# Attention and two dense layers on one core: two-pass values, factors by DMA, a new order of the engines

## The chip, the cores and the metric

One core of one Trainium2 chip runs the whole program. The metric is the device time of one execution in microseconds. Three runs of the kernel before gave a median of 1122.53 us (1120.88 to 1122.81). Engines are named as in the profile: PE is TensorE, DVE is VectorE, ACT is ScalarE, POOL is GpSimd, SP is the engine that issues the DMAs.

## What is computed

Attention with a memory over 4 batches x 8 heads, 576 positions, 64 columns a head, then two dense layers over the 2304 tokens. All inputs are fp32.

```python
B, H, S, D = q.shape                      # 4, 8, 576, 64
scores = scale * np.matmul(q, k.transpose(0, 1, 3, 2))
scores = np.where(causal, -1000000000.0, scores)
a = np.exp(scores - scores.max(-1, keepdims=True))
a /= a.sum(-1, keepdims=True) + 1e-09
local = np.matmul(a, v)
q_p = phi(q)                              # where(x > 0, x, exp(x) - 1) + 1
mem_ret = np.einsum('bhsd,bhde->bhse', q_p, M_prev)
mem_norm = np.einsum('bhsd,bhd->bhs', q_p, z_prev)[..., None] + 1e-06
g = 1.0 / (1.0 + np.exp(-beta))[None, :, None, None]
attn = g * mem_ret / mem_norm + (1 - g) * local
...
h = x @ w_in;  y = np.where(h > 0, h, np.exp(np.minimum(h, 0)) - 1) @ w_out
h = y @ w_in2; out = (h * np.clip(h + 3, 0, 6) / 6) @ w_out2
```

## The kernel before, in words

**Tiling.** Two heads make a pair; there are 16 pairs. The 576 queries of a head are four tiles of 128 and a last one of 64; the last tiles of both heads share one tile of 128 rows. `scores` (L370) writes the scores of query tile i for both heads, `max_rows` (L730) takes their minimum on DVE (the scores are negated), `exp_rows` (L546) the exponentials with their sums on ACT. The order of tiles is 4, 3, 2, 1, 0 (`ORDER`, L24). Then `turn` (L399) transposes the probabilities on PE in ten chunks: G (the last tile), C00 to C11 (key tiles 0 and 1 of each head), C2, C3, RMAIN (the row factors), PHI and TAIL. The chunks go through a ring of two PSUM banks (`ring_at`, L150; `chunk_free`, L390).

**High and low parts.** Products keep their precision by splitting each fp32 operand into a rounded `fp32r` part and the rest. ACT rounds a chunk (`round_chunk`, L564), DVE subtracts (`split_chunk`, L741) to give `pt_lo`. `times_v` (L439) then multiplies in three passes: high x high, low x high, high x low; the values of each head stand in a 128-column stationary tile in which the other head's 64 columns are zero. `times_m` (L454) adds the memory product for both heads at once, again in three passes. All of it accumulates in one output area (`X_AT`, L153).

**Factors.** The row sums and norms give 1/sum and the gate (`row_stats` L781 on DVE, `factors` L325 on POOL). The attention factors are laid over all partitions by nine broadcast transposes (L428, L436), copied by ACT into `r_rows` (L570, L591, L592), and `store_x` (L791) multiplies the output by them on DVE. The memory factors scale `phi` on POOL (`scale_phi` L335). `phi` of q is made in two DVE steps (L771, L774) and one exponential on ACT.

**Order.** Each engine has an order written out by hand as a loop over g (L501, L646, L830): the scores of pair g are interleaved with the turns of pair g-1. Counting semaphores are shared by all tasks of a kind (`pt_lo_done`, `pv_done`, `turned`), so that a wait counts positions in that order. `load_qk` and `load_nat` on SP bring the inputs two pairs ahead.

**Layers.** A chunk of 384 tokens goes through 16 hidden tiles: `hidden` (L463), the activation (`exp_tile` on ACT, `activate` L804 on DVE), `output` (L477). The weights are rounded on ACT (`hi_weights`) and split on POOL (`lo_weights` L293) during the first chunk. In the kernel before the first hidden tiles are mixed into the last pair (L518), and one weight tile is split in the attention stage.

## Time and profile before

| | before |
|---|---|
| median of three runs | 1122.53 us |
| the profiled execution's own time | 1122.92 us |
| its span, first to last instruction | 1121.1 us |
| PE busy (modelled ends) | 1076.2 us, 96% |
| DVE, ACT, POOL busy | 677.8, 298.4, 192.5 us |
| mean granted clock of PE | 0.993 |

The attention stage takes somewhat more than a quarter of the span, the two layers the rest. The busy shares above are means over both. Ends of matmuls are modelled in the trace, so the distance between starts is the better measure of what one costs. "Granted clock" is the share of full speed that PE was given: 1.0 is 2.4 GHz, 0.5 is 1.2 GHz.

### The profile page before, as it was taken

Reading aid. Unit: us, or ns where it says so; the run is one execution under the profiler, and the core shown is the slowest. Engines: PE = TensorE matmul, PEld = TensorE weight load, DVE = VectorE, ACT = ScalarE, POOL = GpSimd, SP = SyncE. Lnnn points to the kernel's source line nnn. Section 1 sums busy time; section 2 is a strip of 40 time slices with the busy share of each in tenths; the row PEclk is TensorE's granted clock in tenths of the full one; section 3 lists DMA queues with packets and bytes.
Section 4 is the critical chain, followed back from the end, with each engine's and each line's share of the span. In section 5 each row is a group of like instructions: output and inputs, shape, how many; then the busy total and the mean of one; then the engine's idle time right before and its main releaser. Section 6 shows DMA issues by size and latency. Waiting matters only on the chain.

```text
span 1121.1 us, 16386 instructions
## 1 busy us (share of the span) xinstructions
PE 1076.2 (96%) x6080; PEld 966.3 (86%) x6080; DVE 677.8 (60%) x1278; ACT 298.4 (27%) x737; POOL 192.5 (17%) x202
## 2 busy tenths in 40 slices
PE   5999999999889999999999999899999999999998
PEld 2667676676879999999999999898999999899997
DVE  5676766767388544545454468865656565565654
ACT  3666666666432212112121123301001010000100
POOL 3434434344265000000000025500000000000000
PEclk9999999999889999999999999999999999999999
DMA  4322121220134000000000014100000000000000
GB/s 162 119 97 101 52 101 56 98 101 20 38 113 132 1 1 1 0 0 0 0 0 0 0 37 131 57 1 13 15 0 28 0 28 0 0 28 0 28 0 28
DMA packets 16599, 44.56 MB, mean 40 GB/s; under 512 B 1968, under 2 KB 1968, under 8 KB 16560
## 3 DMA queue, kind: packets, MB, share of 16 engines
q1 hardware_dynamic: 16560, 44.05, 11.3%
q8 instruction: 23, 0.38, 0.1%
q14 instruction: 16, 0.13, 0.0%
HBM read 39.33 MB, written 4.72 MB: 39 GB/s over the span
## 4 chain that ended last, share of the span: by engine, by line
PE 89%; DVE 6%; issue 3%; ACT 1%; DMA 1%; SPq 0%; DVEq 0%
PE ps L473 35%; PE ps L494 18%; PE ps L486 17%; PE ps L450 8%; PE ps L384 3%; DVE pt_lo L751 2%; PE ps L379 1%; PE ps L459 1%; PE ps L428 1%; PE ps L418 1%; PE ps L387 1%; DVE x_all L795 1%; ACT r_rows L570 1%; PE ps L405 1%; DVE h_hi L824 1%
## 5 line engine op out<-in xcount | busy, mean ns | idle before, releaser
L473 PE MATMUL ps<-x_hi,w 128*128 128x384 f32 x1536 | 392.5, 336 | 0.0
L473 PEld LDWEIGHTS ps<-x_hi,w 128*128 128x128 f32 x1536 | 280.9, 189 | 7.4
L473 PE MATMUL ps<-x_lo,w 128*128 128x384 f32 x768 | 258.3, 336 | 0.0
L486 PE MATMUL ps<-h_hi,w 128*128 128x384 f32 x768 | 196.6, 336 | 6.0 <-DVE h_lo L826 6.0
L494 PE MATMUL ps<-w,h_hi 128*128 128x512 f32 x576 | 179.2, 392 | 3.1 <-DVE h_lo L826 3.1
L824 DVE CAST h_hi<-act_tmp 128x384 fp32r<-128x384 f32 x192 | 108.9, 567 | 100.9 <-PE ps L486 53.2
L486 PEld LDWEIGHTS ps<-h_hi,w 128*128 128x128 f32 x768 | 139.5, 189 | 7.0 <-DVE h_lo L826 7.0
L473 PEld LDWEIGHTS ps<-x_lo,w 128*128 128x128 f32 x768 | 144.7, 188 | 0.0
L296 POOL TENSOR_TENSOR w<-stage,w 128x1024 f32 (+1 forms) x32 | 77.7, 2436 | 358.3 <-ACT w L544 358.3
L486 PE MATMUL ps<-h_lo,w 128*128 128x384 f32 x384 | 129.0, 336 | 0.0
L494 PEld LDWEIGHTS ps<-w,h_hi 128*128 128x128 f32 x576 | 106.8, 188 | 22.1 <-issue 2.4
L633 ACT ACTIVATE e_act<-ps 128x384 f32<-128x384 f32 x96 | 47.2, 492 | 288.3 <-PE ps L473 288.3
L826 DVE TENSOR_TENSOR h_lo<-act_tmp,h_hi 128x384 fp32r<-128x384 f32 x192 | 113.5, 591 | 6.7
L817 DVE TENSOR_SCALAR act_tmp<-ps 128x384 f32<-128x384 f32 x96 | 53.4, 556 | 99.9 <-PE ps L473 99.9
L494 PE MATMUL ps<-w,h_lo 128*128 128x512 f32 x288 | 113.7, 395 | 0.0
L811 DVE TENSOR_SCALAR act_tmp<-e_act 128x384 f32<-128x384 f32 x96 | 38.8, 404 | 109.7 <-ACT e_act L633 108.3
L610 ACT ACTIVATE x_hi<-x_all 128x384 fp32r (+1 forms) x48 | 21.2, 513 | 300.3 <-PE ps L473 299.9
L560 ACT ACTIVATE prob<-ps,neg_max 128x512 f32<-128x512 f32 (+3 forms) x128 | 66.6, 531 | 24.7 <-DVE neg_max L739 24.7
L486 PEld LDWEIGHTS ps<-h_lo,w 128*128 128x128 f32 x384 | 72.6, 189 | 0.0
L739 DVE TENSOR_REDUCE neg_max<-ps 128x2 f32<-128x1024 f32 (+1 forms) x64 | 52.4, 819 | 32.3 <-PE ps L387 32.2
L450 PE MATMUL ps<-pt_hi,v_hi 128*128 128x128 f32 (+2 forms) x192 | 63.8, 332 | 2.9 <-DVE x_all L795 2.9
L494 PEld LDWEIGHTS ps<-w,h_lo 128*128 128x128 f32 x288 | 54.0, 187 | 11.5
(110 smaller groups left out, 1233.8 us busy)
## 6 DMA issues: line engine op xcount, KB each, us to landing
nat<-nat_in SPq DMA_DIRECT2D x16, 768.0 KB, 5.4
qk<-qk_t SPq DMA_DIRECT2D x16, 608.0 KB, 3.8
stage<-w_in SPq DMA_DIRECT2D x32, 256.0 KB, 2.7
stage<-w_out SPq DMA_DIRECT2D x32, 256.0 KB, 2.9
out<-rows_out SPq DMA_DIRECT2D x18, 256.0 KB, 2.1
beta_sb<-beta SPq DMA_DIRECT2D x1, 4.0 KB, 6.5
```

Source lines behind the costliest of these rows:

```text
L296: pool.tensor_tensor(tile[:, 1], stage[:, r], tile.bitcast(F32)[:, 0], ALU.subtract).then_inc(w_split, 1)
L450: mm = pe.matmul(ps[:, X_AT + lo:X_AT + hi], v_tile(v, u, a, t), blocks(pt, a, t, lo, hi), start=(a == 0 and t == 0 and part == 0), stop=F ...
L473: mm = pe.matmul(ps[:, bank:bank + CHUNK], w[:, n, wp, 0, cols], xp[:, m, :], start=(m == 0 and part == 0), stop=(m == KM - 1 and part == 2))
L486: mm = pe.matmul(ps[:, Y_AT + 512 * m:Y_AT + 512 * m + CHUNK], w[:, n, wp, 1, cols], hp[:, n % 2, :], start=(n == 0 and part == 0), stop=( ...
L494: mm = pe.matmul(ps[:, Y_AT + 512 * m:Y_AT + 512 * m + DM], hp[:, n % 2, rows], w[:, n, wp, 1, :], start=(n == 0 and part == 0), stop=(n = ...
L560: ex = act.activation(rows_of(u, i, a), ps[:, at:at + WIDTH[i]], ACT.Exp, bias=neg_max[:, u, x:x + 1], scale=-1.0, accum_out=stats[:, u, x ...
L633: act.activation(e_act[:, n % 2, :], ps[:, 512 * (n % 4):512 * (n % 4) + CHUNK], ACT.Exp).then_inc(h_exp_done, 1)
L739: dve.tensor_reduce(neg_max[:, u, 2 * i:2 * i + 2], rows, AX_X, ALU.min).then_inc(max_done, 1)
L811: dve.tensor_scalar(tmp, e_act[:, n % 2, :], 1.0, -1.0, ALU.min, ALU.add).then_inc(e_free, 1)
L817: dve.tensor_scalar(tmp, h, 3.0, 0.0, ALU.add, ALU.max).then_inc(act_step, 1)
L824: dve.tensor_copy(h_hi[:, n % 2, :], tmp).then_inc(h_hi_done, 1)
L826: dve.tensor_tensor(h_lo[:, n % 2, :], tmp, h_hi.bitcast(F32)[:, n % 2, :], ALU.subtract).then_inc(h_split, 1)
```

## The change

The attention stage is rewritten; the loops of the layers stay as they are, but for the start of the first chunk.

- **Values and memory in two passes.** The stationary tile of a head now holds the high part of its values in 64 columns and the low part in the other 64 (`v_split`, `m_split`), and it is multiplied with `pt_hi` and `pt_lo`. The output rows 0 to 63 and 64 to 127 are then two partial results of one head, each head has a bank of its own (`x_at`), and the first 128 queries have a bank in the ring (Q0, `first_rows`). ACT copies the lower partial results to SBUF (`low_rows`, `low_first`), DVE adds them to the upper ones into `x_all` (`sum_x`, `sum_first`), POOL multiplies by the factors (`store_x`).
- **Factors.** One transpose of a 9-column tile, one small ACT copy, a DMA to a DRAM buffer and four DMAs that load it back broadcast over 64 partitions each.
- **Phi** of q is the larger of q + 1 (now on POOL, `phi_line`) and min(exp q, 1) (DVE); one DVE step goes.
- **Semaphores:** one for each kind of task (`scored[i]`, `low_done[c]`, `rounded[c]`, `turned[c]`, `pv_done[t]`).
- **A new order on all engines** over g, with the pairs in the order of batches. The last pair's chunks use the banks of the scores (`LAST_BANKS`). Three weight tiles are rounded and split during the attention stage, and `nat` and `phi_exp` move to where the layers' tiles lie.

The diff, cut to its core:

```diff
+G, C00, C01, C10, C11, C2, R, C3, PHI, TAIL = range(10)
+Q0 = 10
+RING = (G, Q0, C00, C01, C10, R, C11, C2, C3, PHI, TAIL)
+LAST_BANKS = {C00: 5, C01: 0, C10: 1, C11: 2, C2: 3, C3: 4, R: 3, PHI: 5, TAIL: 2}
+LAST_BEFORE = {C00: G, C3: Q0, R: C2, PHI: C00, TAIL: C11, Q0: C3}
...
+            def spread_r(p):
+                sp.wait_ge(rounded[R], p + 1)
+                sp.dma_start(r_dram[p % 2], r_turned[0:2 * FULL + 1, :]).then_inc(r_sent, 16)
+                sp.wait_ge(r_sent, 16 * (p + 1))
+                if p >= 1:
+                    sp.wait_ge(x_stored, p)
+                for a in range(2):
+                    main = r_dram[p % 2, FULL * a:FULL * a + FULL].rearrange("i q -> (i q)").rearrange("(o x) -> o x", o=1)
+                    tail = r_dram[p % 2, 2 * FULL:2 * FULL + 1, REST * a:REST * a + REST]
+                    sp.dma_start(r_rows[D * a:D * a + D, 0:EDGE], main.to_broadcast([D, EDGE])).then_inc(r_loaded, 16)
+                    sp.dma_start(r_rows[D * a:D * a + D, EDGE:S], tail.to_broadcast([D, REST])).then_inc(r_loaded, 16)
...
+            for g in range(3, PAIRS + 4):
+                if is_pair(g - 4):
+                    spread_r(g - 4)
+                if 9 <= g < 9 + EARLY:
+                    load_weights(g - 9 + STAGES)
+                if is_pair(g - 1):
+                    load_qk(g - 1)
+                    load_nat(g - 1)
...
+            def store_x(p):
+                at = x_all_at(p)
+                x = x_all[:, at:at + S]
+                pool.wait_ge(x_summed, p + 1)
+                pool.wait_ge(q0_summed, p + 1)
+                pool.wait_ge(r_loaded, 64 * (p + 1))
+                pool.tensor_tensor(x, x, r_rows[:, :], ALU.mult).then_inc(x_stored, 1)
...
+            for g in range(2, PAIRS + 3):
+                if is_pair(g - 6):
+                    store_x(g - 6)
+                if is_pair(g - 5):
+                    scale_phi(g - 5)
+                if is_pair(g - 3):
+                    phi_line(g - 3)
+                if is_pair(g - 4):
+                    low_vm(g - 4)
+                if is_pair(g - 3):
+                    phi_by_z(g - 3)
+                if 5 <= g < 5 + EARLY:
+                    lo_weights(w[:, g - 5], g - 5, g - 5)
+                if is_pair(g - 2) and g >= 3:
+                    scale_q(g - 2)
+                if is_pair(g - 3):
+                    round_vm(g - 3)
+                if is_pair(g - 4):
+                    factors(g - 4)
+            scale_phi(PAIRS - 2)
+            low_vm(PAIRS - 1)
+            store_x(PAIRS - 3)
+            factors(PAIRS - 1)
+            scale_phi(PAIRS - 1)
+            lo_weights(w[:, EARLY], EARLY, EARLY)
+            store_x(PAIRS - 2)
+            store_x(PAIRS - 1)
...
+                elif c == R:
                     pe.wait_ge(r_ready, p + 1)
...
+                    mm = pe.transpose(ps[0:2 * FULL + 1, at:at + P], r_nat[:, u, 0:2 * FULL + 1], ident[:, :])
...
+            def first_values(p, a):
+                u = p % 2
+                if a == 0:
+                    pe.wait_ge(low_done[C00], p + 1)
                     pe.wait_ge(vm_split, p + 1)
                     if p >= 1:
...
+                        pe.wait_ge(x_summed, p)
+                else:
+                    pe.wait_ge(low_done[C01], p + 1)
+                for part, pt in enumerate((pt_hi, pt_lo)):
+                    mm = pe.matmul(ps[:, x_at(a):x_at(a) + S - P], v_tile(u, a, 0), blocks(pt, a, 0, P, S), start=(part == 0), stop=False)
+                mm.then_inc(pv_done[0], 1)
+            def times_v(p, t):
+                u = p % 2
+                if t < LAST:
+                    pe.wait_ge(low_done[(C11, C2, C3)[t - 1]], p + 1)
                 for a in range(2):
...
+                    for part, pt in enumerate((pt_hi, pt_lo)):
+                        mm = pe.matmul(ps[:, x_at(a) + P * t - P:x_at(a) + S - P], v_tile(u, a, t), blocks(pt, a, t, P * t, S), start=False, stop=False)
+                mm.then_inc(pv_done[t], 1)
             def times_m(p):
                 u = p % 2
...
+                pe.wait_ge(low_done[TAIL], p + 1)
+                for part, ph in enumerate((phi_t_hi, phi_t_lo)):
+                    for a in range(2):
+                        d = slice(D * a, D * a + D)
+                        mm = pe.matmul(ps[:, x_at(a):x_at(a) + S - P], m_tile(u, a)[d], ph[d, P:S], start=False, stop=(part == 1))
+                mm.then_inc(memory_done, 1)
+            def first_rows(p):
+                u, at = p % 2, ring_at(p + 1, Q0)
+                chunk_free(p + 1, Q0)
+                for a in range(2):
+                    for part, pt in enumerate((pt_hi, pt_lo)):
+                        pe.matmul(ps[:, at + P * a:at + P * a + P], v_tile(u, a, 0), blocks(pt, a, 0, 0, P),
+                                  start=(a == 0 and part == 0), stop=False)
+                for part, ph in enumerate((phi_t_hi, phi_t_lo)):
+                    for a in range(2):
+                        mm = pe.matmul(ps[:, at + P * a:at + P * a + P], m_tile(u, a), ph[:, 0:P], start=False, stop=(a == 1 and part == 1))
+                mm.then_inc(q0_done, 1)
...
+            for g in range(2, PAIRS + 2):
+                if is_pair(g - 3):
+                    turn(g - 3, G)
+                    scores(g - 3, 0)
+                if is_pair(g - 4):
+                    times_m(g - 4)
+                if is_pair(g - 2):
+                    scores(g - 2, 4)
+                if is_pair(g - 4):
+                    first_rows(g - 4)
+                if is_pair(g - 3):
+                    turn(g - 3, C00)
+                if is_pair(g - 2):
+                    scores(g - 2, 3)
+                if is_pair(g - 3):
+                    turn(g - 3, C01)
+                    turn(g - 3, C10)
+                if is_pair(g - 2):
+                    scores(g - 2, 2)
+                if is_pair(g - 3):
+                    first_values(g - 3, 0)
+                    first_values(g - 3, 1)
+                    turn(g - 3, R)
+                    turn(g - 3, C11)
+                if is_pair(g - 2):
+                    scores(g - 2, 1)
+                if is_pair(g - 3):
+                    turn(g - 3, C2)
+                    turn(g - 3, C3)
+                if is_pair(g - 3):
+                    times_v(g - 3, 1)
+                    turn(g - 3, PHI)
+                    times_v(g - 3, 2)
+                    turn(g - 3, TAIL)
+                    times_v(g - 3, 3)
+                    times_v(g - 3, 4)
+            last = PAIRS - 1
+            turn(last, G)
+            scores(last, 0)
+            times_m(last - 1)
+            first_rows(last - 1)
+            turn(last, C00)
+            turn(last, C01)
+            turn(last, C10)
+            turn(last, C11)
+            turn(last, C2)
+            first_values(last, 0)
+            turn(last, C3)
+            first_values(last, 1)
+            times_v(last, 1)
+            turn(last, R)
+            turn(last, PHI)
+            times_v(last, 2)
+            turn(last, TAIL)
+            pe.wait_ge(low_done[C01], PAIRS)
+            hidden(0, 0, 0)
+            times_v(last, 3)
+            times_v(last, 4)
+            pe.wait_ge(low_done[C10], PAIRS)
+            hidden(0, 1, 0)
+            times_m(last)
+            first_rows(last)
+            pe.wait_ge(low_done[TAIL], PAIRS)
+            hidden(0, 2, 0)
...
+            def low_rows(p):
+                act.wait_ge(memory_done, p + 1)
+                heads = ps[D:P, x_at(0):x_at(0) + 1024].rearrange("p (a q) -> p a q", a=2)
+                act.activation(x_low[D:P, :, P:S], heads[:, :, 0:S - P], ACT.Copy).then_inc(x_low_done, 1)
+            def low_first(p):
+                at = ring_at(p + 1, Q0)
+                act.wait_ge(q0_done, p + 1)
+                act.activation(x_low[D:P, :, 0:P], ps[D:P, at:at + 2 * P].rearrange("p (a q) -> p a q", a=2), ACT.Copy).then_inc(q0_low_done, 1)
...
+            def sum_x(p):
+                at = x_all_at(p)
+                dve.wait_ge(x_low_done, p + 1)
+                for a in range(2):
+                    add = dve.tensor_tensor(x_all[D * a:D * a + D, at + P:at + S], ps[0:D, x_at(a):x_at(a) + S - P], x_low[D:P, a, P:S], ALU.add)
+                add.then_inc(x_summed, 1)
+            def sum_first(p):
+                at, q0 = x_all_at(p), ring_at(p + 1, Q0)
+                dve.wait_ge(q0_low_done, p + 1)
+                for a in range(2):
+                    add = dve.tensor_tensor(x_all[D * a:D * a + D, at:at + P], ps[0:D, q0 + P * a:q0 + P * a + P], x_low[D:P, a, 0:P], ALU.add)
+                add.then_inc(q0_summed, 1)
...
+            max_rows(0, 4)
+            max_rows(0, 3)
+            gates()
             phi_of_q(0)
...
+            for g in range(2, PAIRS + 2):
+                if is_pair(g - 4):
+                    sum_first(g - 4)
+                if is_pair(g - 3):
+                    split_chunk(g - 3, C00)
+                if is_pair(g - 2) and g >= 3:
+                    max_rows(g - 2, 3)
+                if is_pair(g - 3):
+                    row_stats(g - 3)
+                    split_chunk(g - 3, C01)
+                    split_chunk(g - 3, C10)
+                if is_pair(g - 2):
+                    max_rows(g - 2, 2)
+                if is_pair(g - 3):
+                    split_chunk(g - 3, C11)
+                if is_pair(g - 2):
+                    max_rows(g - 2, 1)
+                if is_pair(g - 3):
+                    split_chunk(g - 3, C2)
+                    split_chunk(g - 3, C3)
+                if is_pair(g - 3):
+                    split_chunk(g - 3, PHI)
+                if is_pair(g - 2):
+                    norms(g - 2)
+                if is_pair(g - 3):
+                    split_chunk(g - 3, TAIL)
+                if is_pair(g - 1):
+                    phi_of_q(g - 1)
+                if is_pair(g - 2):
+                    max_rows(g - 2, 0)
+                    split_chunk(g - 2, G)
+                if is_pair(g - 1):
+                    max_rows(g - 1, 4)
+                if is_pair(g - 3):
+                    sum_x(g - 3)
+            last = PAIRS - 1
+            sum_first(last - 1)
+            dve.sem_inc(h_free, 4)
+            dve.sem_inc(e_free, 2)
+            dve.sem_inc(hidden_used, 2)
+            split_chunk(last, C00)
+            row_stats(last)
+            split_chunk(last, C01)
+            split_chunk(last, C10)
+            split_chunk(last, C11)
+            split_chunk(last, C2)
+            split_chunk(last, C3)
+            x_rest(0, 0)
+            split_chunk(last, PHI)
+            split_chunk(last, TAIL)
+            activate(0, 0, 0)
+            sum_x(last)
+            sum_first(last)
+            dve.wait_ge(x_summed, PAIRS)
+            dve.wait_ge(q0_summed, PAIRS)
+            dve.sem_inc(y_free, KM)
```

## Rows read from the trace of the kernel before

**Rows 1.** Busy time by stage, one pair: window, PE, PEld, DVE, ACT, POOL, clock, DMA

```profile
162.90:180.40 17.50, 16.37 (x112) 12.17 (x112) 11.98 (x23) 11.07 (x32) 6.96 (x10) 1.00 0.24 86
```

**Rows 2.** Chain of waits, a steady pair, then the first layer: start, us, what

```profile
58.10 0.99 PE ps L379 x4
...
59.68 0.59 PE ps L450 x6
...
60.27 1.04 PE ps L459 x6
...
61.31 1.06 PE ps L384 x4
...
64.47 1.22 DVE pt_lo L751 x2
...
66.50 2.12 PE ps L450 x12
...
70.24 1.22 PE ps L450 x6
...
72.10 0.89 PE ps L428 x8
...
73.01 0.61 ACT r_rows L570
...
74.10 1.52 PE ps L450 x12
...
75.62 0.51 PE ps L379 x2
...
325.12 2.08 PE ps L473 x12
```

**Rows 3.** Groups of instructions by shape, twelve steady pairs: busy us, mean ns, idle before

```profile
L751 DVE TENSOR_TENSOR pt_lo<-ps,pt_hi 128x384 fp32r<-128x384 f32 x24 | 12.1, 546 | 0.0
...
L795 DVE TENSOR_TENSOR x_all<-ps,r_rows 128x576 f32<-128x576 f32 x12 | 9.0, 747 | 0.0
...
L771 DVE TENSOR_SCALAR phi<-nat 128x640 f32<-128x640 f32 x13 | 6.4, 495 | 31.4 <-PE ps L436 31.4
...
L774 DVE SCALAR_TENSOR_TENSOR phi<-phi_exp,phi 128x640 f32<-128x640 f32 x12 | 9.9, 826 | 0.4
...
L339 POOL TENSOR_TENSOR phi<-phi,f_nat 128x640 f32<-128x640 f32 x12 | 15.1, 1259 | 0.9
...
L315 POOL TENSOR_TENSOR v_lo<-nat,v_hi 128x640 fp32r<-128x640 f32 x12 | 18.7, 1561 | 0.0
...
L301 POOL TENSOR_SCALAR qk<-qk 128x640 f32<-128x640 f32 x12 | 8.7, 728 | 0.0
```

**Rows 4.** DMA issues by line: count, KB each, median us to landing

```profile
beta_sb<-beta SPq DMA_DIRECT2D x1, 4.0 KB, 6.5
```

**Rows 5.** Instructions in order of time, start of kernel: start, us, engine, line

```profile
5.15 2.26 PE L379 MATMUL ps<-qk 128*128 128x288 f32 x4 [5.15 <-POOL qk L301]
...
15.11 0.76 DVE L735 TENSOR_REDUCE neg_max<-ps 128x1 f32<-128x576 f32 x1
...
24.53 0.46 PE L405 MATMUL ps<-ident,prob 128*128 128x128 f32 x1
```

**Rows 6.** Instructions in order of time, last pair; then busy time by stage

```profile
285.50 0.27 PE L405 MATMUL ps<-ident,prob 128*128 128x128 f32 x1
...
315.19 0.69 PE L486 MATMUL ps<-h_hi,w 128*128 128x384 f32 x1 [4.87 <-DVE h_lo L826]
...
322.75 0.44 PE L486 MATMUL ps<-h_hi,w 128*128 128x384 f32 x1 [0.27 <-DVE h_lo L826]
...
315.00:320.00 5.00, 4.80 (x15) 4.81 (x16) 4.93 (x4) 0.90 (x1) 5.00 (x3) 0.50 0.54 190
```

**Rows 7.** Instructions in order of time, the gates and the first values split

```profile
13.52 1.53 POOL L315 TENSOR_TENSOR v_lo<-nat,v_hi 128x640 fp32r<-128x640 f32 x1
...
13.63 1.44 DVE L728 COPY rest_by<-rest 64x4 f32<-64x4 f32 x1
```

More of the change, by code:

```diff
@@ L406, in turn @@
                 elif c in (C00, C01, C10, C11):
-                    if c == C00:
-                        pe.wait_ge(exp_done, QT * p + QT)
+                    if c in (C00, C01):
+                        pe.wait_ge(exp_done[0], 2 * p + (1 if c == C00 else 2))
                     a, t = (c - C00) % 2, (c - C00) // 2
@@ L439, in times_v @@
             def times_v(p, t):
                 u = p % 2
-                pe.wait_ge(pt_lo_done, LOS * p + LO_RANK[(C01, C11, C2, C3, C3)[t]] + 1)
-                if t == 0:
-                    pe.wait_ge(vm_split, p + 1)
-                    if p >= 1:
-                        pe.wait_ge(x_stored, p)
-                cuts = (0, X_CUT, S) if t == 0 else (P * t, S)
-                for a in range(2):
-                    for lo, hi in zip(cuts, cuts[1:]):
-                        for part, (v, pt) in enumerate(((v_hi, pt_hi), (v_lo, pt_hi), (v_hi, pt_lo))):
-                            mm = pe.matmul(ps[:, X_AT + lo:X_AT + hi], v_tile(v, u, a, t), blocks(pt, a, t, lo, hi),
-                                           start=(a == 0 and t == 0 and part == 0), stop=False)
@@ new lines, in _ @@
+            last = PAIRS - 1
+            round_chunk(last - 1, C2)
+            round_chunk(last - 1, C3)
+            exp_rows(last, 2, 1)
+            round_chunk(last - 1, PHI)
+            exp_rows(last, 1, 0)
+            round_chunk(last - 1, TAIL)
+            exp_rows(last, 1, 1)
+            round_chunk(last, G)
+            low_rows(last - 1)
+            exp_rows(last, 0, 0)
+            exp_rows(last, 0, 1)
+            low_first(last - 1)
+            round_chunk(last, C00)
+            round_chunk(last, C01)
@@ new lines, in _ @@
+            round_chunk(last, C10)
+            round_chunk(last, C11)
+            round_chunk(last, C2)
+            round_chunk(last, C3)
+            act.wait_ge(scored[0], PAIRS)
+            act.wait_ge(phi_done, PAIRS)
+            x_round(0, 0)
+            round_chunk(last, R)
+            round_chunk(last, PHI)
+            round_chunk(last, TAIL)
+            act.wait_ge(vm_split, PAIRS)
+            act.wait_ge(phi_z_done, PAIRS)
+            hi_weights(EARLY)
+            exp_tile(0, 0)
@@ L668, in _ @@
+            low_rows(last)
+            low_first(last)
+            for n in range(EARLY + 1, SOON):
+                hi_weights(n)
+                exp_tile(0, n - EARLY)
             act.wait_ge(x_stored, PAIRS)
-            act.sem_inc(y_free, KM)
-            hi_weights(EARLY)
-            hi_weights(EARLY + 1)
-            for n in range(1, KF):
+            hi_weights(SOON)
+            for n in range(SOON - EARLY, KF):
                 exp_tile(0, n)
@@ new lines, in _ @@
+            last = PAIRS - 1
+            sum_first(last - 1)
[12 more added lines that the diff above has]
+            split_chunk(last, TAIL)
@@ L856, in _ @@
+            activate(0, 0, 0)
[4 more added lines that the diff above has]
+            dve.sem_inc(y_free, KM)
+            for n in range(1, KF):
                 activate(0, n, 0)
```

430 lines of the change are left out of this document (198 added, 232 removed).

## The prediction

> **What bounds the kernel now.** The first view is the profile's busy line by stage: in one attention period TensorE's modelled busy time is 16.37 of 17.50 us, VectorE's 11.98, ScalarE's 11.07, GpSimd's 6.96 [rows 1]. A high TensorE share alone doesn't tell whether it works or waits, so I read the chain of waits over one period next [rows 2]. It repeats: the scores of the padded last tile start at 58.10 and again at 75.62, so a pair of heads costs 17.52 us, and 16 pairs make about 280 us of the 1121.1 us span. The chain is TensorE's own work but for two stretches: from 64.47 to 66.50 it runs through VectorE (the row statistics before, two `pt_lo` splits, then the store of `x_all` that frees the output bank), and again at 73.01 through ScalarE's copy of the factor rows. The behind-the-attention rest (the two layers, 384 groups of 2.08 us, a row of which is the last in [rows 2]) is TensorE without gaps, and the diff leaves its loops alone. So the question is the period, and the two ends of the attention stage.
>
> TensorE's own work in a period: 4.5 us from 58.10 to 62.6, the end of the score at 61.31 and its two masks (scores of the last tile and of tile 3, G, the last values, the memory product), 6.5 us between 66.50 and the end of the factor turns at 72.99, 1.96 us from the tail turns to 75.62, and 2.6 us that the chain leaves out (14 turns of 0.11 us and one score of 384 columns with its mask, 1.07 us by its neighbours). That is 15.55 us, and 1.97 us of waiting.
>
> **The change, part by part.** *Two passes instead of three for values and memory.* Prices per matmul come from the chain [rows 2]: 448 columns 1.22/6 = 0.203 us; the 320 and 192 columns 1.52/12 = 0.127 us; 64 columns 0.59/6 = 0.098 us; 128 columns 0.11 us (0.89/8). Before: 0.59 + 1.04 + 2.12 + 1.22 + 1.52 = 6.49 us. After: the first key tile 4 x 0.203 = 0.81; the second the same 0.81; third and fourth 8 x 0.127 = 1.01; the last 4 x 0.098 = 0.39; the memory product 4 x 0.203 = 0.81; the first 128 rows in a bank of their own 8 x 0.111 = 0.89. Sum 4.72, so -1.77 us.
>
> *Factors spread by DMA.* Nine broadcast turns become one: 8 x 0.111 = -0.89 us on TensorE [rows 2], and ScalarE's three copies become one small one. TensorE's work falls by 2.66 us to 12.9 us a period.
>
> The 64-row memory products could be cheaper still. In this trace four 64-row score matmuls of 512 columns take 1.06 us, while four 128-row ones of 288 columns take 0.99 us [rows 2]: 0.52 against 0.86 ns a column, so the two heads, which lie on different rows of the array, overlap at least in part. The bounds of the new memory product are thus 0.4 and 0.81 us, and I take 0.81, because the `fp32r` rows near it have no 64-row case. The Trainium skill, "TensorE: Matmul & The Clock Gate", section Part 3: Packing small matmuls, says that matmuls on different row groups run at once; by it the sum would hold 0.4 us less a period, and the trace's score rows agree.
>
> *What is added elsewhere.* VectorE [rows 3]: it loses the store (0.747) and the first half of phi (0.495), and gains two sums of 64 x 448 (each between 0.546 for 384 columns and 0.747 for 576, I take 0.62) and two of 128 columns (by the same two rows 1.05 ns a column, so 0.28 each): 11.98 - 1.24 + 1.80 = 12.5 us. ScalarE loses a copy of 512 columns (0.61 in [rows 2]) and two small ones (0.4 together, an estimate from it), and gains a copy of 896 columns (between 0.61 and twice that; I take 0.9), one of 256 (0.4) and a small one (0.25): 11.6 us. GpSimd gains the store's product (576 columns: 1.13 to 1.4 by the 1.259 and 1.561 us of its 640-column rows), the line of phi (0.728) and two small factor products (0.2 each, no more than a third of the smallest row here): 6.96 + 2.4 = 9.4 us, and in three periods a weight split more (1024 columns at the rate of the 1.561 row: 2.5 us), with a ScalarE rounding.
>
> So three engines stand close: TensorE 12.9, VectorE 12.5, ScalarE 11.6. The period can't be under 12.9 us, and what it is above that depends on hand-overs.
>
> *The new order.* I walked one period of the new order by hand with these durations (a hand-over costs the full duration of the giver). TensorE waits in three places. The second head's first values need the low part of chunk C01, which VectorE reaches after a maximum of 512 columns and the row statistics: about 0.6 us. The phi turn needs the bank of C2, which goes ScalarE 0.61, VectorE 0.61 (1.22/2) after the turn, against 0.81 us of values in between: about 0.3 us. C3 needs C11's bank: 0.1 us. Everything else arrives early: the wait for the store of before (ahead of 66.50 in [rows 2]) is now on the sum of the pair before, which VectorE does ahead of C00; the factor copy's wait at 73.01 is gone, since nothing on TensorE waits for the spread. The reciprocals' consumer, GpSimd, waits at the statistics with about 3 us of slack, so its port is free there. Period: 12.9 + 1.0 = 13.9 us. VectorE is busy 12.5 of them, with 1.4 us spare, so it is nearly the second bound.
>
> *Queues.* On SP the spread adds one store, a wait for its landing, a wait for the store of the pair before, and four broadcast loads, ahead of the loads of `qk` and `nat`. A small broadcast at the start, behind larger loads, took 6.5 us to land [rows 4], which I take as the upper bound of each; two of them are 13 us and the lower bound is nothing; the consumer on GpSimd comes about 13 us after the turn. What is queued behind it, the load of `qk` for three pairs on, could not start earlier than its own wait on the scores in any case. I cost it at nothing; if the cover goes, it is GpSimd's store that is late, and behind it the scaling of phi.
>
> *The start.* Before, VectorE does the gates first: its first maximum is at 15.11 and the G turn of pair 0 at 24.53 [rows 5]. After, two maxima come first, as soon as the scores are there (5.15 + 2.26). By hand: exponentials to 12.4, gates 12.6 to 14.7, phi of pair 0 at 15.5, then a wait for GpSimd's line of pair 1 until 19.6. The place in the order that corresponds to G(0) is 18.9: -5.6 us.
>
> *The end.* From G of the last pair to output 1 of the first chunk it is 285.50 to 322.75, 37.3 us [rows 6]. Of that, TensorE waits 4.9 us before 315.19, and from 315 to 320 the granted clock is 0.50, the level of 1.2 GHz. After: the last pair's chunks have banks of their own, the first three weight tiles are already split, and three hidden groups come between the last values. TensorE's own work there is 31 turns 3.4, scores 0.6, products of pair 14 1.7 and of pair 15 4.7, four hidden groups and one output at 2.08 [rows 2] 10.4, sum 20.8 us. By hand it waits about 2.2 us (for VectorE's splits and the x split at the first hidden group, and for the second hidden tile's low part). 23.0 us: -14.3. No wait is as long as the 4.9 us after which the clock was low, so I take the high level throughout.
>
> **The sum**, on the profiled run (1121.1 span, 1122.9 with what lies around it, which is 0.4 above the median 1122.5): G(0) at 18.9; G(15) at 18.9 + 15 x 13.9 = 227.4; output 1 at 250.4; the rest as before, 1121.1 - 322.75 = 798.35, gives 1048.8; plus 1.8 around it 1050.6. Predicted 1050 us.
>
> **The rivals.**
> *A. VectorE becomes the bound, by GpSimd's port.* In [rows 7] a 64 x 4 copy on VectorE takes 1.44 us because GpSimd's 1.53 us operation started just before it. GpSimd is now busy 9.4 of 13.9 us instead of 7 of 17.5. If phi's product on VectorE (0.826 in [rows 3], two SBUF inputs) always falls behind `v_lo` (1.561), the period is 12.5 + 1.56 and the hand-overs' 0.9: 15.0; with the statistics behind a 1.26 us operation too, 15.3. For it: the rows. Against: in my walk GpSimd waits at both places. The Trainium skill, "SBUF — State Buffer", section Who interferes with whom, gives the rule: the pair of ports shared by VectorE and GpSimd is locked for a whole instruction, and a VectorE instruction with two SBUF inputs meets it while one with a PSUM input doesn't; the trace agrees with 1.44 us. Time: 1050 + 15 x 1.1 to 1.4 = 1067 to 1071.
> *B. The waits stay.* The old order waited 1.97 us a pair; if the new one does too, the period is 14.9 and the time 1065.
> *C. The 64-row products overlap* (0.4 each, and C01 comes earlier): period 13.5, time 1044. With the waits gone as well 12.9, time 1035.
> *D. The end doesn't shorten* by more than its three prepared tiles (30 us instead of 23): 1057.
> *E. Slower than before: the spread's round trip.* The loop is: factor turn, round trip, store on GpSimd (1.4), scaling of phi (1.26), phi turn, and 10.7 us later the factor turn of two pairs on. The period is then (round trip + 13.9)/2. It rules from a round trip of 13.9 us on; to be slower than before, the period must be over 18.6, so the round trip over 23 us. At 26 us the time is 1050 + 15 x 6 = 1140. Against it: no DMA that small landed later than 6.5 us [rows 4].
> *F. The change does not do what it says*: TensorE's 2.66 us a pair are really issued less, so only the hand-overs could eat them; with 17.5 us of period kept, only the ends would give 20 us: 1103.
>
> **How the numbers follow.** Forecast (period 13.6 to 14.3) 0.48; C 0.17; A and B 0.25; D 0.05; F 0.02; E 0.02; smaller than 12.9 a period, which would need a price above to be too high, 0.01. The range reaches from C with no waits, 1036, to A with both blocks, 1073. What a measurement of this kernel can tell from no change is about 0.2%, 2 us. Faster by more 0.97, within 0.01, slower 0.02.
>
> **What would show it.** The distance between two equal places of the chain: 13.9 us (15 if A or B). VectorE's busy time 12.5 a period; phi's product at 0.83 us in all pairs, and 1.5 or more under A. TensorE's waits before the second first-values matmul and the phi turn. G(15) near 227 us, output 1 of the first chunk near 250, and 798 us behind it. GpSimd's store waiting for the spread would speak for E. Wrong would be most of all: a clock at the lower level in the attention stage, or operations on 64 partitions priced unlike 128.

## The result, and the profile after

The changed kernel takes 1078.4 us (median of 4, 1075.9 to 1080.2) against 1121.7 us (1120.3 to 1122.8): ratio 0.961, 95% interval 0.959 to 0.964. The forecast was 1050, its range 1036 to 1073. So the change is faster, but it gives 43 us where 72 were forecast. The profiled run's span is 1076.6 us, its mean granted clock 0.993.

The busy line of one steady pair, which answers to [rows 1] (window, PE, PEld, DVE, ACT, POOL, clock, DMA):

```profile
160.65:175.96 15.31, 14.21 (x94) 9.61 (x94) 13.59 (x25) 11.58 (x33) 9.30 (x15) 1.00 0.32 107
```

A pair takes 15.31 us, not 13.9. ScalarE and GpSimd are busy as forecast (11.6 and 9.4); VectorE is at 13.59 instead of 12.5. The groups by shape over twelve pairs, answering to [rows 3], show which line holds the difference:

```profile
L984 DVE SCALAR_TENSOR_TENSOR phi<-phi_exp,phi 128x640 f32<-128x640 f32 x12 | 24.7, 2062 | 0.0
...
L404 POOL TENSOR_SCALAR phi<-nat 128x640 f32<-128x640 f32 x12 | 8.7, 723 | 27.7 <-PE ps L521 27.7
L1005 DVE TENSOR_TENSOR x_all<-ps,x_low 64x448 f32<-64x448 f32 x22 | 13.6, 617 | 0.5
...
L1012 DVE TENSOR_TENSOR x_all<-ps,x_low 64x128 f32<-64x128 f32 x22 | 6.2, 283 | 0.5
```

Phi's product took 0.826 us before and takes 2.06; that is the 1.24 us. The two sums cost what they were priced at. The idle time of GpSimd's line of phi (L404) is put down to TensorE's L521, the tail turn. One pair in order of time (start, us, engine, line, and the idle time before it with its end):

```profile
171.12 0.27 PE L521 MATMUL ps<-ident,phi 128*128 128x128 f32 x1
...
171.56 0.72 POOL L404 TENSOR_SCALAR phi<-nat 128x640 f32<-128x640 f32 x1 [2.32 <-PE ps L521]
...
172.66 1.55 POOL L360 TENSOR_TENSOR v_split<-nat,v_split 128x640 fp32r<-128x640 f32 x1
...
172.82 2.07 DVE L984 SCALAR_TENSOR_TENSOR phi<-phi_exp,phi 128x640 f32<-128x640 f32 x1
```

GpSimd waits 2.32 us until TensorE has turned the last tile of phi of two pairs before, since phi has two buffers. The low part of the values (L360) stands behind that wait and so starts 0.16 us before phi's product, which ends 0.68 us after it.

TensorE meets the delay later in VectorE's order. The bank for the turn of C01 is free once VectorE has added up the first 128 queries of the pair before (L1012), and the turn waits 0.56 us for it:

```profile
163.10 1.27 PE L503 MATMUL ps<-ident,prob 128*128 128x128 f32 x7 [0.56 <-DVE x_all L1012]
```

The spread, for [rows 4]: its DMAs land 2.5 to 2.6 us after issue (count, KB each, median us).

```profile
r_rows<-r_dram SPq DMA_DIRECT2D x32, 128.0 KB, 2.6
r_rows<-r_dram SPq DMA_DIRECT2D x32, 16.0 KB, 2.5
```

The ends, for [rows 5] and [rows 6]: G of the last pair, GpSimd's splits, output tile 1 and output tile 2 of the first chunk.

```profile
248.68 0.66 PE L495 MATMUL ps<-ident,prob 128*128 128x128 f32 x4
...
269.80 12.70 POOL L339 TENSOR_TENSOR w<-stage,w 128x1024 f32 x5
...
272.77 0.62 PE L591 MATMUL ps<-h_hi,w 128*128 128x384 f32 x2 [0.93 <-DVE h_lo L1044]
...
280.33 0.97 PE L591 MATMUL ps<-h_hi,w 128*128 128x384 f32 x2 [3.12 <-DVE h_lo L1044]
```

The chain of waits there (start, us, what) and the clock (the last number but two of a busy line):

```profile
268.46 1.60 DVE h_hi L1042
...
270.09 2.62 DVE h_lo L1044
272.71 2.49 DVE act_tmp L1029
...
275.23 0.57 DVE act_tmp L1031
...
275.82 1.84 DVE h_hi L1042
...
277.68 2.60 DVE h_lo L1044
...
280.33 3.91 PE ps L591 x12
284.24 2.08 PE ps L578 x12
...
281.00:282.00 1.00, 1.00 (x4) 1.00 (x4) 1.00 (x1) 0.00 (x0) 1.00 (x1) 0.50 1.02 293
```

While GpSimd does five splits at a stretch (12.7 us), the steps of VectorE shown here that have all their inputs in SBUF take 1.8 to 2.6 us (the one of 1.60 stands beside GpSimd's store just before); L1031, which has one input in PSUM, stays at 0.57. TensorE waits 3.12 us for them, and the next output runs mostly at clock 0.50, the level of 1.2 GHz (281 to 283): 3.91 us instead of 2.08.

### The profile page after: what moved, and what is told of

It is laid out like the page before. It is cut to its first block, busy times and chain, and to the rows that moved or that the text cites. A ratio compares the mean times of both kernels' runs of the same rounds, so it can differ in the third digit from the quotient of the medians.

```text
span 1076.6 us, 15983 instructions
## 1 busy us (share of the span) xinstructions
PE 1037.4 (96%) x5792; PEld 921.7 (86%) x5792; DVE 696.7 (65%) x1309; ACT 306.1 (28%) x737; POOL 228.5 (21%) x265
## 4 chain that ended last, share of the span: by engine, by line
PE 79%; DVE 16%; ACT 3%; issue 1%; DMA 0%; POOL 0%; ACTq 0%; DVEq 0%
PE ps L578 36%; PE ps L599 19%; PE ps L591 18%; DVE phi L984 3%; DVE neg_max L955 2%; DVE pt_lo L965 2%; DVE x_all L1005 2%; PE ps L464 1%; DVE pt_lo L968 1%; PE ps L519 1%; DVE phi_t_lo L974 1%; PE ps L534 1%; DVE neg_max L951 1%; ACT pt_hi L744 1%; ACT phi_t_hi L748 1%
## 5 line engine op out<-in xcount | busy, mean ns | idle before, releaser
L1042 DVE CAST h_hi<-act_tmp 128x384 fp32r<-128x384 f32 x192 | 109.1, 568 | 101.3 <-PE ps L591 52.5
L1044 DVE TENSOR_TENSOR h_lo<-act_tmp,h_hi 128x384 fp32r<-128x384 f32 x192 | 113.4, 591 | 6.7
L1029 DVE TENSOR_SCALAR act_tmp<-e_act 128x384 f32<-128x384 f32 x96 | 39.6, 413 | 112.7 <-ACT e_act L790 111.3
L767 ACT ACTIVATE x_hi<-x_all 128x384 fp32r (+1 forms) x48 | 21.2, 514 | 300.2 <-PE ps L578 300.2
L464 PE MATMUL ps<-qk 64*128 64x512 f32 (+3 forms) x256 | 54.5, 504 | 4.8 <-ACT prob L712 4.8
L1039 DVE TENSOR_TENSOR act_tmp<-ps,act_tmp 128x384 f32<-128x384 f32 x96 | 53.5, 558 | 3.3
```

Of the source, the lines that this page charges most:

```text
L464: pe.matmul(ps[:, at:at + WIDTH[i]], qk[d, u, P * i:P * i + P], qk[d, u, QCOLS:QCOLS + WIDTH[i]], start=True, stop=False)
L1029: dve.tensor_scalar(tmp, e_act[:, n % 2, :], 1.0, -1.0, ALU.min, ALU.add).then_inc(e_free, 1)
L1039: dve.tensor_tensor(tmp, h, tmp, ALU.mult).then_inc(h_free, 1)
L1042: dve.tensor_copy(h_hi[:, n % 2, :], tmp).then_inc(h_hi_done, 1)
L1044: dve.tensor_tensor(h_lo[:, n % 2, :], tmp, h_hi.bitcast(F32)[:, n % 2, :], ALU.subtract).then_inc(h_split, 1)
```

## The experiments

Each was timed in three rounds beside the kernel before on the same chip. The main theory at first: the miss in the period is the collision of phi's product with GpSimd.

**e1_low_first**: the low parts go ahead of the line of phi.

```
-                if is_pair(g - 3):
-                    phi_line(g - 3)
                 if is_pair(g - 4):
                     low_vm(g - 4)
+                if is_pair(g - 3):
+                    phi_line(g - 3)
```

> Edit: on GpSimd the low parts of the values (low_vm) come before the line of phi (phi_line). In the changed kernel phi_line waits for the turn of TAIL, and the 1.55 us low part behind it runs while VectorE wants to make phi's product, which then takes 2.07 instead of 0.83 us in 14 of 16 pairs. Theory 1 (the shared port is what lengthens the period): the low part now runs during GpSimd's wait, phi's product falls to 0.83 us, the period from 15.3 to about 14.1 us, and the time by 15 x 1.24 = 19 us, to 1060 us. Theory 2 (VectorE's order and its hand-overs set the period, and the product's length only fills a gap it would have had): the product is short, the period stays 15.2 to 15.3, time 1076 to 1079 us. Theory 3 (TensorE's own work and waits): the same as theory 2.

Measured: 1072.1 us (ratio 0.956, 0.954 to 0.958); phi's product is back at 0.816 us, and the period is 14.84. So the collision is real, but it is worth 0.47 us a pair, a third of the 1.41 that were missing, and neither theory's time came out. TensorE's weight load for the turn of C01 waits 0.25 us for L1012 instead of 0.73, the same half microsecond. (The 6.3 us of the time are not 15 such periods: the second G turn comes 2.4 us later than in the changed kernel, 36.17 against 33.73, and the end of the stage gives back 2.4.) The chain of waits over one period shows what stands in its place:

```profile
163.99 0.28 DVE inv L999
164.27 0.56 DVE pt_lo L965
164.83 0.04 issue
164.87 0.67 PE ps L534 x2
...
167.31 0.61 ACT pt_hi L744
167.92 0.02 issue
167.94 0.70 DVE pt_lo L968
168.65 0.04 issue
168.69 0.66 PE ps L519 x4
...
172.06 0.60 PE ps L552 x4
172.66 1.17 PE ps L459 x4
...
173.90 0.76 DVE neg_max L951
174.65 0.03 issue
174.69 0.62 DVE x_all L1005
...
177.18 1.22 DVE neg_max L955
```

It goes round: VectorE's maximum of the last tile (173.90), the sums of the pair before, C00, a maximum, the row statistics, C01 (to 164.83 in the period shown first), 5.8 us; then TensorE's second first values (164.87) to the end of the next last-tile scores (173.83), 9.0 us, with one trip through ScalarE and VectorE (C2) in it.

**e2_pe_less**: the second pass, `pt_lo`, is left out for key tiles 1 to 3; nothing else changes.

```
-                    for part, pt in enumerate((pt_hi, pt_lo)):
+                    for part, pt in enumerate((pt_hi, pt_lo) if t == LAST else (pt_hi,)):
```

> Leaves out part of the computation: the second pass (with the low parts of the probabilities) over key tiles 1 to 3, six matmuls or 0.91 us of TensorE's work a pair. Theory 1 and 2 (VectorE's chain with the port is the bound, TensorE waits): the period falls by less than 0.3 us, the time by 0 to 4 us, 1074 to 1078 us. Theory 3 (TensorE's work counts, as in the prediction, which began its sum with 12.9 us of it): 15 x 0.9 = 13.5 us less, 1065 us.

Measured: 1072.5 us (0.957, 0.955 to 0.959), period 15.02. Of 0.91 us of TensorE work 0.29 came back, the period that theories 1 and 2 had; the time is 1.5 us below their range. Phi's product fell to 1.77 us beside it: the tail turn comes earlier, and the low part on GpSimd starts 0.46 us before the product, not 0.16.

**e3_norms_short**: the norm sums (L989) over one tile of five; the other four are left out.

> Leaves out part of the computation: the sums of the memory norms are taken for one of five query tiles only, VectorE's reduction falls from 0.81 to about 0.3 us a pair. It stands just ahead of phi's product in VectorE's order. Theory 1 (who starts first takes the port): the product would start about 0.5 us earlier, beside or ahead of the 1.55 us low part on GpSimd, and falls to between 0.83 and 1.3 us: 1.3 to 1.8 us a period, 20 to 27 us in all, 1051 to 1058 us, far more than the 0.5 us taken out. Rival (the end of the product is fixed by the low part, whichever of them comes first): 0 us, 1078. Theory 2 (VectorE's work is the bound, the port doesn't matter): 15 x 0.5 = 8 us, 1070 us.

Measured: 1071.2 us (0.955, 0.953 to 0.957), period 14.83, phi's product 0.826: with the sums shorter the product comes just before GpSimd's operation, and it is that one which waits (2.20 us instead of 1.55):

```profile
168.62 0.83 DVE L984 SCALAR_TENSOR_TENSOR phi<-phi_exp,phi 128x640 f32<-128x640 f32 x1 [0.25 <-ACT phi_exp L758]
168.66 2.20 POOL L360 TENSOR_TENSOR v_split<-nat,v_split 128x640 fp32r<-128x640 f32 x1
```

So this run removed the collision too, and ends at the same period as e1_low_first; the 1051 to 1058 us of theory 1 missed. The low part of the values is ready 2.2 us after the product's start here (170.86 and 168.62) and 1.6 us before it in e1_low_first (169.84 and 171.48), so it isn't an earlier low part that helped there.

**e4_end_out**: the low parts of the weight tiles 4 to 15 of the first layer are split in 8 columns of their rows only (the rest of that work is left out, ScalarE fills the place).

> Leaves out part of the computation: the low parts of the weight tiles 4 to 15 of the first layer are not split on GpSimd (8 columns instead of 1024; ScalarE writes the place instead). In the changed kernel GpSimd does five of these splits back to back from 269.8 to 282.5 us, VectorE's steps on SBUF take 2.5 us each beside them, TensorE waits 0.9 and 3.1 us and then runs 3 us at the lower clock. Theory (the port costs the end 5 us): VectorE's steps take 0.36 and 0.56 us, no wait of TensorE over 1 us after output 0, the clock stays at its high level, 5 to 6 us less: 1072 to 1074 us. Rival (the second hidden tile is late for another reason, ScalarE's exponential behind the weight roundings): 0 to 1 us, 1077 to 1078 us.

Measured: 1071.2 us (0.955, 0.954 to 0.957), period 15.31 as it was. The stretch after output 0 is without gaps and at full clock:

```profile
264.44 2.17 PE ps L580 x12
266.62 2.15 PE ps L593 x12
268.77 2.08 PE ps L580 x12
...
270.00:280.00 10.00, 10.00 (x59) 10.00 (x59) 5.62 (x13) 7.03 (x10) 1.02 (x3) 1.00 0.65 216
```

From the last pair's reciprocal to output 3 it is 31.6 us in the changed kernel (254.56 to 286.16) and 25.4 here (253.58 to 279.01). So the splits cost 6.2 us in this stretch, by way of VectorE; of the rest of the 7.2 about 1.0 lies at the start of the kernel, where the edit does nothing (the second G turn is at 32.70 instead of 33.73).

**e5_low_pe_less**: e1_low_first and e2_pe_less together.

> The order of GpSimd is that of e1_low_first, and the second pass (the low part of the probabilities) over key tiles 1 to 3 is left out as in e2_pe_less: 0.91 us less TensorE work a pair. Loop theory: in e1_low_first a pair takes 14.84 us because of a loop that is half VectorE (maximum of the last tile, sums, C00, a maximum, row statistics, C01) and half TensorE (first values, C11, scores, values of tiles 1 to 4, G, scores, memory product, scores of the last tile). Of the 0.91 us, 0.29 (tile 1) and 0.22 (tile 3) lie on the loop, the 0.4 of tile 2 lie in a wait for the phi turn: period 14.33, time 1064.5. Rival: VectorE alone bounds the pair (busy 12.6 of 14.84, the rest waits for ScalarE and GpSimd): period stays 14.84, time 1072.

Measured: 1071.6 us (0.957, 0.954 to 0.959), period 14.82: a miss for the loop as I had written it, since 0.9 us less TensorE work give nothing. But VectorE alone isn't the bound either, as the chain shows what closes the loop now:

```profile
166.19 0.61 ACT pt_hi L744
...
166.82 0.70 DVE pt_lo L968
...
167.56 0.67 PE ps L519 x4
...
168.26 0.61 ACT phi_t_hi L748
...
168.89 0.70 DVE phi_t_lo L974
...
169.63 0.66 PE ps L495 x4
```

C2's bank must be free for the phi turn, and phi's for the next G turn (L495). From the start of the phi turn to G (167.56 to 169.63) that is 2.07 us of hand-overs, and in e1_low_first it is 2.07 us of TensorE's work (168.69 to 170.76). Ahead of the phi turn both have the same trip of C2, 1.4 us. Two paths of the same length: shortening one changes nothing.

**e6_low_stats**: the row statistics behind C01, and on TensorE the scores of tile 1 ahead of the turns of R and C11.

```
+                    split_chunk(g - 3, C01)
                     row_stats(g - 3)
-                    split_chunk(g - 3, C01)
```

> The order of GpSimd is that of e1_low_first; on top VectorE does the row statistics behind C01 instead of ahead of it, and TensorE the scores of tile 1 ahead of the turns of R and C11. Loop theory: 0.68 us of row statistics leave the loop, period 14.2, time 1062 to 1063. Rival, VectorE alone bounds the pair: its work is the same in another order, period 14.84, time 1072.

Measured: 1074.9 us (0.958, 0.957 to 0.960), period 14.97. Both theories missed. In the trace the chain now runs from VectorE's maximum of tile 3 through ScalarE's exponentials to the scores of tile 1, and C11, which stands behind them, is what the next values wait for: the second half of the edit cost what the first gained.

**e7_low_end**: one weight split ahead of the last pair's store, its rounding ahead of ScalarE's copies of the last pair.

```
             store_x(PAIRS - 2)
+            lo_weights(w[:, STAGES], STAGES, 0)
             store_x(PAIRS - 1)
```

> The order of GpSimd is that of e1_low_first; on top the end of the attention stage is changed and nothing is left out: ScalarE rounds the fifth weight tile before it copies the last pair's low partial results, and GpSimd splits it before the last pair's store instead of behind it, and its loop over groups begins one group later. Theory of the end (after output 1 GpSimd owes five weight splits of 2.5 us at a stretch, TensorE starves and its clock falls): one split leaves the stretch, 3 to 5 of the 7.2 us that e4_end_out showed come back, time 1067 to 1069. Rival: what was gained in e4_end_out was the low clock alone, which one split less doesn't avoid: 1071 to 1072.

Measured: 1071.2 us (0.955, 0.953 to 0.957), 0.9 us under e1_low_first, which the ranges of the two runs (1070.9 to 1071.3, 1070.8 to 1073.5) don't separate; the 3 to 5 us that were expected missed. The split that was moved blocks VectorE's `h_lo` (2.62 us) where it stands now, and three more follow the store. Moving one doesn't take it away from VectorE. The clock explains nothing here: it stays at 1.00 from 262 to 282, as it did behind output 1 in e1_low_first.

**e8_low_stats_sum_end**: e6 and e7 together, and the sum of the pair before ahead of the maximum of the last tile on VectorE.

```
+                if is_pair(g - 3):
+                    sum_x(g - 3)
                 if is_pair(g - 1):
                     max_rows(g - 1, 4)
-                if is_pair(g - 3):
-                    sum_x(g - 3)
```

> Everything together and nothing left out: GpSimd's order of e1_low_first, the statistics behind C01 of e6_low_stats, the sum of the pair before ahead of the maximum of the last tile (VectorE waits less for ScalarE's copy there, 0.25 us a pair at most), and the end of e7_low_end. Loop theory: period 13.9 to 14.2, time 1053 to 1059. Rival, VectorE alone bounds the pair: 1067 to 1072 by the end alone.

Measured: 1068.6 us (0.953, 0.952 to 0.955), period 14.60: against e6_low_stats the sum gave 0.37 us a pair, while the statistics, with the scores moved, had cost 0.13 there, which is why the time stays above the 1053 to 1059 of the loop theory.

That left a clean question, work as a whole or work on the loop. The next two take nearly the same 0.5 us from VectorE, once on the loop and once beside it.

**e9_low_max_short**: e1_low_first, and the last tile's maximum over 64 of 576 columns.

```
-                    ... ps[:, at:at + S], AX_X, ALU.min).then_inc(max_done[LAST], 1)
+                    ... ps[:, at:at + D], AX_X, ALU.min).then_inc(max_done[LAST], 1)
```

> GpSimd's order of e1_low_first; the maximum of the last tile (one row maximum of 576 columns on VectorE) is taken over 64 of its columns only, so the rest of that maximum is left out: about 0.5 us less VectorE work a pair, and these 0.5 us lie between TensorE's scores of the last tile and C01's low part. Loop theory in its second form: the loop has one half on VectorE (maximum of the last tile to C01), and its other half is closed by two paths of nearly the same length, TensorE's own work (14.84 us a pair in e1_low_first) and the bank hand-overs C2, PHI, G, each through ScalarE and VectorE (14.82 in e5_low_pe_less, where the work was cut and the period stayed). So a cut in VectorE's half shortens both: period 14.3, time 1064. Rival (VectorE's work as a whole bounds, wherever it lies): also 14.3. Rival (TensorE and the hand-overs bound by themselves): 14.84, 1072.

**e10_low_norms_short**: e1_low_first and e3_norms_short together.

> GpSimd's order of e1_low_first; the norm sums are taken for one tile of five, the other four are left out, as in e3_norms_short: 0.5 us less VectorE work a pair, and these lie outside the loop, between the splits of PHI and TAIL, ahead of a wait of VectorE for the scores. Loop theory: period unchanged, 14.84 us, time 1072. Rival (VectorE's work as a whole bounds): 14.3, 1064, the same as e9_low_max_short.

Measured: e9 has a period of 14.30 and 1066.1 us (0.950, 0.949 to 0.952); e10 one of 14.83 and 1071.7 us (0.956, 0.954 to 0.958). The groups by shape of the two, e9's line first:

```profile
L951 DVE TENSOR_REDUCE neg_max<-ps 128x1 f32<-128x64 f32 x12 | 2.7, 225 | 8.1 <-PE ps L460 8.1
```

```profile
L989 DVE TENSOR_REDUCE stats<-phi_z 128x2 f32<-128x128 f32 x12 | 3.3, 276 | 0.0
```

0.53 us each (0.758 to 0.225, 0.809 to 0.276). On the loop they shorten the pair by 0.54 (14.84 to 14.30), beside it by nothing. That excludes VectorE's work as a whole, and TensorE with the hand-overs by themselves.

**e11_low_sum_end**: the sum early as in e8, the statistics where they were, the end of e7. Nothing is left out.

> Nothing left out: GpSimd's order of e1_low_first, the end of e7_low_end, and VectorE sums the pair before ahead of the maximum of the last tile, not behind it. In e1_low_first VectorE waits 0.67 us for that tile's scores and then has 1.25 us of sum in the loop; ScalarE's copy is done about 1.0 us before. Loop theory: of the sum 0.3 to 0.4 us fit into the wait, period 14.45 to 14.55, time 1065 to 1067 (e8_low_stats_sum_end, with the statistics moved as well, had 14.60 and 1068.6). Rival (the same work in another order changes nothing): 14.84 and 1071.

Measured: 1065.9 us (0.951, 0.950 to 0.953), period 14.46. This is the fastest version that computes everything: 12.5 us under the change. What it gains over e7 is about 15 times 0.37 us, by the order of two operations.

**e12_three_phi**: a third buffer for phi, so that the line of phi waits for the tail turn of three pairs before, not of two; the order is untouched.

```
-                if p >= 2:
-                    pool.wait_ge(turned[TAIL], p - 1)
+                if p >= 3:
+                    pool.wait_ge(turned[TAIL], p - 2)
```

> Nothing left out and no order changed: phi gets a third buffer, so GpSimd's line of phi waits for the tail turn of three pairs before instead of two. Theory of the port: that wait alone put the low parts of the values beside phi's product on VectorE. Without it the product takes 0.83 us again and the period is that of e1_low_first, 14.8 to 14.9, time 1070 to 1073. Rival (what helped in e1_low_first was the earlier low part of the values, which the first values wait for): the product may stay at 2 us and the period at 15.3, time 1078.

Measured: 1069.2 us (0.954, 0.952 to 0.956), period 14.83, phi's product 0.816. The buffer alone does to the period what the order did in e1, so the wait on the tail turn is the cause of the collision.

## Why the prediction was wrong, point by point

The misses add up to the difference. The profiled run takes 1076.6 + 1.8 = 1078.4 us against the sum of 1050.6, 27.8 more: the start 0.1, the period 15 x 1.41 = 21.2, the end to output 1 1.1, what follows 5.5 (803.8 us from 272.77 to the end, against 798.35).

- **The start was right.** G(15) at 248.68 less 15 x 15.31 is 19.0, against 18.9, and phi's product of pair 1, from which the 18.9 was read, starts at 19.27, against 19.6. (18.9 is a place in the order, not a turn: the G turn of pair 0 starts at 13.37, that of pair 1 at 33.73, that of pair 2 15.9 us later; from there the pairs take 15.3.)
- **"Against: in my walk GpSimd waits at both places" failed for one of the two, and with it the case against rival A.** At the statistics GpSimd does wait, 2.50 us in the pair shown (about 3 in the walk), and they run undelayed. At phi's product it doesn't, and the sum put that collision at nothing. I had overlooked one line of the diff: `phi_line` waits for `turned[TAIL]` of two pairs before. It holds GpSimd 2.3 us, and what is queued behind it, the low part of the values, lands on the product. Rival A named this pair of operations. That its 15.3 is also the number measured (15.31) is luck: it needed the statistics delayed too, and a period bounded by VectorE. It priced the block at 1.56 us; the product got 1.24 us longer, and the runs give 0.47 us of period to it (e1, e3, e12). The row of 1.44 us on which rival A leaned is a copy with one SBUF input; it shows one operation held up by another, not what two SBUF inputs or a PSUM input do. The Trainium skill, "SBUF — State Buffer", section Who interferes with whom, has the lock of the port pair shared by VectorE and GpSimd last for a whole instruction and, outside the two-port modes, spares a VectorE instruction with at most one input in SBUF; the trace agrees with 2.07 us for the product and 0.57 us for L1031 beside GpSimd's splits.
- **"Period: 12.9 + 1.0 = 13.9 us" was 0.93 us short, even without the collision (e1: 14.84).** The walk summed TensorE's work and three waits; what closes is a loop, 5.8 us on VectorE and 9.0 us on TensorE, and e9 shows that its VectorE half counts in full. By the distances between TensorE's starts in e1 (155.94 to 170.76) the wait before the second first values is 0.55 us (0.6 in the walk) and that before the phi turn 0.42 (0.3). But "everything else arrives early" failed: the turns of C01 and C10 wait for VectorE's sums and for C00's low part, and take 1.20 us for 7 x 0.11. The weight loads of these turns show the two waits:

```profile
161.77 0.42 PEld L503 LDWEIGHTS ps<-ident,prob 128*128 128x128 f32 x4 [0.25 <-DVE x_all L1012]
162.49 0.31 PEld L503 LDWEIGHTS ps<-ident,prob 128*128 128x128 f32 x3 [0.30 <-DVE pt_lo L965]
```

Along the chain the same 0.93 us look otherwise. The "issue" pieces of 0.01 to 0.04 us at each hand-over sum to 0.3 a period. And TensorE's two stretches in it each begin with matmuls that take longer there than the distance between starts by which I priced them: the two first values 0.67 against 2 x 0.203, the phi turn 0.66 against 4 x 0.111, 0.48 together. That these are most of it is worked out from rows and wasn't tested.
- **The prices of TensorE's work were right but for one.** The memory product is 0.60 us a pair in the chain of e1, not 0.81: rival C's overlap is there, by half of its bound. Its gain probably didn't reach the period, as the 0.91 us that e5 left out didn't.
- **VectorE's, ScalarE's and GpSimd's prices were right**: 0.617 and 0.283 us for the sums (0.62, 0.28), 11.58 and 9.30 us busy (11.6, 9.4). 12.5 us for VectorE holds once the product's 1.24 us are taken off (12.35; 12.45 in e1).
- **The spread costs nothing in 15 of 16 pairs, as said; rival E is false.** Its loads land in 2.6 us, and GpSimd waits for them only once, for the last pair. There they are issued from 263.94 on, behind the store of the pair before (262.32 to 263.87), and GpSimd's last store starts at 268.41, 1.2 us after its sum is there; the five splits stand behind it. What these 1.2 us cost wasn't tested.
- **The end to output 1 was right**: 248.68 to 272.77 is 24.1 us against 23.0. Rival D is false.
- **"The rest as before" failed by 5.5 us.** The step took the rest from output 1 on, while GpSimd still owed the splits that it had put off: five at a stretch, and beside them the four steps of VectorE for one hidden tile take 7.6 us (272.71 to 280.28) instead of 1.9 (284.22 to 286.15). TensorE's wait of 3.12 us and the 1.83 us that output 2 takes longer at the low clock are 4.95 of the 5.5. "No wait is as long as the 4.9 us" held to the letter, but "so I take the high level throughout" failed: the clock is at 0.50 from 281 to 283 behind the shorter wait. In e1_low_first, where outputs 2 and 3 come with waits of 2.15 and 1.09 us, it stays at 1.00, and from the last reciprocal to output 3 it is 29.2 us instead of 31.6 (25.4 in e4). The trace of before had shown the cause: its wait of 4.87 us [rows 6] ends with VectorE's `h_lo`, which takes 2.73 us beside four splits of GpSimd, and 0.56 us once they are done.

```profile
312.38 9.90 POOL L296 TENSOR_TENSOR w<-stage,w 128x1024 fp32r<-128x1024 f32 x4 [15.27 <-ACT w L544]
312.41 2.73 DVE L826 TENSOR_TENSOR h_lo<-act_tmp,h_hi 128x384 fp32r<-128x384 f32 x1
```

- **Rival B's period of 14.9 us** is what is left once the collision is gone (14.83). A and B were priced as two ways; they came one on top of the other, and their common chance of 0.25 was too small.

## What to carry to other kernels

Where several engines are within some 10% of each other, don't add the waits to the work of the fullest one: follow one hand-over round until it comes back to its own engine one period later, adding for each hand-over of TensorE what its result comes later than the distance between its starts says, and look for a second path of the same length before you price a cut. Read every wait in a moved helper, and for each ask what is queued behind it and beside which operation of the engine that shares the port it will now run. Work that is put off past the end of your sum is still work: find who does it and whom it blocks.

## What the runs showed of the hardware

- Phi's product, a VectorE instruction with two inputs in SBUF, takes 2.06 us instead of 0.82 when a GpSimd instruction of 1.55 us has started 0.16 us before it. In e3, where the product is first, it is GpSimd's that takes 2.20.
- Beside five GpSimd instructions of 2.5 us back to back, VectorE's L1029, L1042 (one SBUF input each) and L1044 (two) take 1.8 to 2.6 us instead of 0.36 to 0.57, about one of them for each of GpSimd's. Not all are held up: L1031, with one input in PSUM, keeps 0.57, and the norm sums (L989), a reduction from SBUF, keep 0.81 beside GpSimd's L404 (171.97 and 171.56 in the changed kernel).
- A wait of 3.12 us, behind one of 0.93 us, came before TensorE's granted clock fell from 1.0 to 0.50 (281 to 283); waits of 2.15 and 1.09 us in e1 didn't bring it down.
- Four 64-row matmuls of 448 columns on two halves of the array take 0.60 us; four 128-row ones of 448 columns are 0.81 by the price from [rows 2]. The halves overlap only in part.
